# Hash attention, a dense layer and eight experts in one kernel: who stores the late rows, where some steps of the first route stand, and a one-hot made in halves

## The reference

```python
def _moe2_ref(x, w_gate, w1, w2):          # x: 1536 tokens x 512; 8 experts, hidden size 1024
    cap = N // E                           # 192 tokens for each expert
    logits = x @ w_gate
    flat = logits.flatten()
    order = np.argsort(-flat)
    for idx in order:
        tok, e = (int(idx) // E, int(idx) % E)
        if assigned[tok] >= 0 or counts[e] >= cap:
            continue
        assigned[tok] = e
        counts[e] += 1
    for e in range(E):
        mask = assigned == e
        h = np.maximum(x[mask] @ w1[e], 0.0)
        out[mask] = h @ w2[e]
```

## Time and profile before

| | us |
|---|---|
| median of 3 runs | 779.58 (777.39 to 780.97) |
| the profiled execution | 779.81 |
| its span | 778.1 |
| around the span | 1.7 |
| mean granted clock of TensorE | 0.993 of full |

### The profile page before, as it was taken

One profiled execution on the slowest core, in us unless ns is written; L12 is line 12 of the kernel. 1 busy time (PEld: TensorE's weight loads), 2 busy tenths in 40 slices (PEclk: granted clock), 3 DMA queues, 4 the chain that ended last, 5 costly groups with the idle time before them and its releaser, 6 DMA issues. The chain is left out here.

```text
span 778.1 us, 13713 instructions
## 1 busy us (share of the span) xinstructions
PE 763.2 (98%) x4537; PEld 693.0 (89%) x4537; DVE 441.7 (57%) x1103; ACT 392.7 (50%) x695; POOL 397.3 (51%) x326
## 2 busy tenths in 40 slices
PE   8999999999999999999999999999899999999996
PEld 6889898988988899999999999997699999999996
DVE  8576666756664348768766667645554455454000
ACT  3677767777676655665665666540112122122221
POOL 5677777777687587576567777530110020011111
PEclk9999999999999999999999999999799999999999
DMA  7676667666536020010010001000644645464731
GB/s 162 145 174 149 144 160 172 143 142 155 149 77 184 1 109 0 0 42 0 0 42 1 0 0 41 1 1 29 228 150 137 230 154 177 186 231 161 250 130 42
DMA packets 44548, 83.61 MB, mean 107 GB/s; under 512 B 17256, under 2 KB 17256, under 8 KB 43728
## 3 DMA queue, kind: packets, MB, share of 16 engines
q1 hardware_dynamic: 42288, 76.68, 35.0%
q0 software_dynamic: 2048, 6.29, 2.4%
q10 hardware_dynamic: 160, 0.00, 0.0%
HBM read 56.64 MB, written 6.29 MB: 81 GB/s over the span
## 5 line engine op out<-in xcount | busy, mean ns | idle before, releaser
L361 POOL TENSOR_TENSOR pt_lo<-pt,pt_hi 128x768 fp32r<-128x768 f32 x64 | 117.7, 1844 | 51.6 <-ACT pt_hi L498 44.2
L995 PE MATMUL banks<-xt_hi,split_parts 128*128 128x384 f32 (+1 forms) x512 | 141.2, 337 | 0.2 <-POOL split_parts L1019 0.2
L1019 POOL TENSOR_TENSOR split_parts<-w_in_sb,split_parts 128x512 fp32r<-128x512 f32 x64 | 84.5, 1320 | 73.8 <-ACT split_parts L1012 72.6
L491 ACT ACTIVATE pt<-banks 128x768 f32<-128x768 f32 x96 | 78.1, 813 | 65.7 <-PE banks L768 55.4
L1384 PE MATMUL banks<-split_parts,h_hi 128*128 128x512 f32 x342 | 106.6, 392 | 0.0
L612 DVE TENSOR_REDUCE mx<-banks 128x1 f32<-128x768 f32 x96 | 90.5, 957 | 23.0 <-PE banks L796 19.0
L995 PEld LDWEIGHTS banks<-xt_hi,split_parts 128*128 128x128 f32 x512 | 93.5, 188 | 3.7 <-issue 0.9
L1961 PE MATMUL banks<-x_cols,w_in_sb 128*128 128x192 f32 x512 | 95.3, 339 | 0.0
L1975 PE MATMUL banks<-expert_hidden,w_out_sb 128*128 128x192 f32 x512 | 92.2, 332 | 0.0
L1961 PEld LDWEIGHTS banks<-x_cols,w_in_sb 128*128 128x128 f32 x512 | 84.7, 196 | 2.3 <-issue 0.8
L995 PE MATMUL banks<-xt_lo,split_parts 128*128 128x384 f32 (+1 forms) x256 | 86.1, 336 | 0.0
(11 more groups left out here) (282 smaller groups left out, 1452.1 us busy)
## 6 DMA issues: line engine op xcount, KB each, us to landing
w_out_sb<-in_moe_w SPq DMA_DIRECT2D x8, 2048.0 KB, 9.5
w_in_sb<-in_moe_w SPq DMA_DIRECT2D x7, 2048.0 KB
w_in_sb<-in_moe_w_in SPq DMA_DIRECT2D x8, 512.0 KB, 6.7
w_out_sb<-in_moe_w_out SPq DMA_DIRECT2D x8, 512.0 KB, 5.3
w_out_sb<-in_k SPq DMA_DIRECT2D x16, 192.0 KB, 3.9
w_out_sb<-in_q SPq DMA_DIRECT2D x16, 192.0 KB, 4.0
v_raw<-in_v SPq DMA_DIRECT2D x16, 192.0 KB, 3.7
ka<-split_parts SPq DMA_DIRECT2D x16, 192.0 KB, 3.0
```

The costliest lines, as they stand in the source:

```text
L361: pool.tensor_tensor(pt_lo[x % 2][:], pt[j % 2][:], pt_hi[x % 2][:].bitcast(fp32), ALU.subtract).then_inc(los, 1)
L491: act.activation(halves(pt[j % 2]), both(ST), ACT.Exp, scale=SCALE).then_inc(ex, 1)
L995: last = pe.matmul(PB[i][:, 0:HALF], w_[:, k, :], x_[:, xs], start=n == 0, stop=n == 3 * DT - 1)
L1019: pool.tensor_tensor(wil[i], in_view(f), wih[i].bitcast(fp32), ALU.subtract).then_inc(wils, 1)
```

## The change

- The three late tiles are stored by ScalarE itself, from its own DMA queue, right behind the eviction of each; SyncE no longer issues them.
- In the route, two steps of VectorE (the ties in `members_and_ties`, and the first update of `waiting`) move from ahead of the counts to behind them; the step on `open_or_filled` moves one place up; `tie_taken` stands beside `slots`, and the second update of `waiting` beside `slot_placed`.
- In route 0 `row_onehot` is made in two halves of six columns each. The first raises `half_list`, the second `asked`, with no drain behind it. TensorE starts on the list with `half_list` and waits for `asked` ahead of its seventh matmul.

```diff
+        w1_rest, half_list = sem("w1_rest"), sem("half_list")
...
-            for t in range(CT):
-                sp.wait_ge(y_tile, t + 1)
-                at = (CHUNKS - 1) * HALF + t * P
-                sp.dma_start(y_rows[at:at + P, :], last_rows[t]).then_inc(stored, 16)
...
                 act.wait_ge(row_tile, t + 1)
                 act.activation(last_rows[t], PB[2 + t][:], ACT.Copy).then_inc(y_tile, 1)
+                act.wait_ge(y_tile, t + 1)
+                at = (CHUNKS - 1) * HALF + t * P
+                act.dma_start(y_rows[at:at + P, :], last_rows[t]).then_inc(stored, 16)
...
                 dve.tensor_tensor(mem[:, 0], mem[:, 0], bgt[:, 1], ALU.add)
-                dve.tensor_tensor(mem[:, 1], bgt[:, 0], bgt[:, 1], ALU.subtract)
-                dve.drain()
-                dve.tensor_tensor(alive[:], alive[:], below[:], ALU.mult)
                 dve.wait_ge(answered, step(2 * NL))
...
+                dve.tensor_tensor(mem[:, 1], bgt[:, 0], bgt[:, 1], ALU.subtract)
+                dve.drain()
+                dve.tensor_reduce(fmax[:], few[:], AX.X, ALU.max)
                 dve.tensor_tensor(cap[:], cap[:], cnt[:, 1], ALU.subtract)
-                dve.drain()
-                dve.tensor_reduce(fmax[:], few[:], AX.X, ALU.max)
+                dve.tensor_tensor(alive[:], alive[:], below[:], ALU.mult)
                 dve.drain()
...
                 dve.tensor_tensor(mem_e[:], mem[:], es[:].unsqueeze(1).unsqueeze(1).broadcast_to([P, 2, NT, E]), ALU.mult)
+                dve.tensor_scalar(openness[:], es[:], -2.0, 1.0, ALU.mult, ALU.add)
                 dve.drain()
                 dve.tensor_reduce(gm[:], mem_e[:], AX.X, ALU.max)
-                dve.tensor_scalar(openness[:], es[:], -2.0, 1.0, ALU.mult, ALU.add)
...
-                dve.drain()
-                rows_and_columns(places)
+                dve.scalar_tensor_tensor(vt[:], places[:, 1], float(CAP), gm[:, 1], ALU.is_lt, ALU.mult)
+                dve.drain()
+                rows_and_columns(True, not past(s, 1))
...
                 dve.drain()
+                if in_halves:
+
+                    dve.tensor_tensor(oh[:, 0:CH, EARLY], row[:, EARLY].unsqueeze(1).broadcast_to([P, CH, NT // 2]),
+                                      iota_j[:, 0:CH, EARLY], ALU.is_equal).then_inc(half_list, 1)
+                    dve.tensor_tensor(oh[:, 0:CH, LATE], row[:, LATE].unsqueeze(1).broadcast_to([P, CH, NT // 2]),
+                                      iota_j[:, 0:CH, LATE], ALU.is_equal).then_inc(asked, 1)
+                    return
...
                 for t in range(NT):
+                    if t == NT // 2 and not past(s, 1):
+                        pe.wait_ge(asked, STEPS)
...
                     pe.wait_ge(first_half, k // 2 + 1)
+                elif k == STEPS - 1 and not past(s, 1):
+                    pe.wait_ge(half_list, 1)
```

More of the change, by code:

```diff
@@ L1559, in experts @@
             sem(n) for n in ("asked", "answered", "e_ready", "list_ready", "w1_in0", "w1_in1", "w2_in0", "w2_in1", "gathered0", "gathered1", "xtp", "xts", "ehid", "ehs", "ecol", "ecs", "erow", "ogs", "scattered", "sp_steps", "psteps", "padded"))
-        w1_rest = sem("w1_rest")
+        w1_rest, half_list = sem("w1_rest"), sem("half_list")
         late_rows, row_tile, last_logits = late
@@ L1782, in route @@
                     dve.scalar_tensor_tensor(few[:], cnt[:, 0], float(CAP), pref[:], ALU.is_ge, ALU.mult)
-                dve.tensor_tensor(cap[:], cap[:], cnt[:, 1], ALU.subtract)
+                dve.tensor_tensor(mem[:, 1], bgt[:, 0], bgt[:, 1], ALU.subtract)
                 dve.drain()
                 dve.tensor_reduce(fmax[:], few[:], AX.X, ALU.max)
+                dve.tensor_tensor(cap[:], cap[:], cnt[:, 1], ALU.subtract)
+                dve.tensor_tensor(alive[:], alive[:], below[:], ALU.mult)
                 dve.drain()
@@ L1805, in route, with rows_and_columns @@
                 dve.scalar_tensor_tensor(slots[:], places, -NOSLOT, gm[:], ALU.add, ALU.mult)
+                dve.scalar_tensor_tensor(vt[:], places[:, 1], float(CAP), gm[:, 1], ALU.is_lt, ALU.mult)
                 dve.drain()
-                rows_and_columns(places)
+                rows_and_columns(True, not past(s, 1))
                 if more:
                     choose()
-            def rows_and_columns(places=None):
+            def rows_and_columns(ties=False, in_halves=False):
                 dve.tensor_tensor(placed[:], slots[:, 0], slots[:, 1], ALU.add)
-                if places is not None:
-                    dve.scalar_tensor_tensor(vt[:], places[:, 1], float(CAP), gm[:, 1], ALU.is_lt, ALU.mult)
+                if ties:
+                    dve.tensor_tensor(alive[:], alive[:], vt[:], ALU.subtract)
                 dve.drain()
@@ L1821, in rows_and_columns @@
                 dve.scalar_tensor_tensor(row[:], back_by[:], NOSLOT, placed[:], ALU.add, ALU.add)
-                if places is not None:
-                    dve.tensor_tensor(alive[:], alive[:], vt[:], ALU.subtract)
                 dve.tensor_tensor(ids_c[:], ids[:].unsqueeze(2).broadcast_to([P, NT, 2, 2]),
```

## The result

| | before | after |
|---|---|---|
| median of 8 runs, us | 778.89 (777.39 to 780.97) | 781.57 (780.82 to 782.39) |
| profiled execution, us | 779.81 | 781.47 |
| its span, us | 778.1 | 779.7 |
| mean granted clock | 0.993 | 0.990 |

The changed kernel is slower: the ratio is 1.0036, with a 95% interval of 1.0023 to 1.005, or 2.7 us by the medians. That is inside the 0.5% that the prediction called no change, but the interval doesn't hold 1, and the forecast was 0.2 us faster. Of all the executions in this document one is slow and left out of its ratio: 837.15 us at a mean granted clock of 0.855, in the first experiment.

A forecast was written before the change was run, and what follows sets the result against it. TensorE, busy 763.2 of 778.1 us, was taken as the bound, with gain only at the layers' switch through VectorE's route 1: 779.81 less 0.24 is 779.57, on the median's footing 779.3 us; range 776.0 to 781.4.

The forecast's parts named there:

- the one on the late rows: Late stores on ScalarE: third lands at 548.7, first weights leave 2.4 us earlier, sum unchanged if it lands by 549.7.
- sharing half and half: Third late store and first weights under way together: equal sharing delays the 2 us store by 1 us at most, to 549.7.
- rival 2: Third late store waits behind the first weights, transposes start at 557.4 instead of 555.58, time 781.4 us; chance 0.10.
- The sentence in the prediction on interleaving: DMA at the late stores: transfers started on several engines interleave on the same 16 DMA engines; only issuing time is saved.
- Nobody waits for these weights: First expert weights on SyncE: issued 2.4 us earlier without gain; before, they landed at 553.0 and expert 0 began at 558.20.
- The slack: Third late store before the gather: it may land 0.65 us later than GpSimd could use it, at 549.7, before delaying transposes.
- ScalarE's issue: Late stores issued by ScalarE: 0.59 us each against SyncE's 0.32, costing nothing since ScalarE idles 2.90 us before `token_list`.
- VectorE's sum: Switch between the layers: VectorE begins route 1 0.24 us earlier, `expert_id` 0.16 us earlier; the 0.24 kept at the transposes.
- every round of that route is a wait of TensorE for VectorE, so nothing in between eats it: Route 1 up to the transposes: VectorE's 0.24 us earlier start arrives there in full.
- What would show it: Signs in the profile after, among them `expert_id` 0.15 us early and transposes directly behind the comparison without idle for the gather.
- Rival 1: Slow stretch around 554 to 566 us: TensorE's clock doesn't fall, saving 3.3 us, time 776.0 us; chance 0.12.
- The longer slow stretch: Around the switch the lower clock lasts longer, each us costing at most 0.36; 5 us more give 781.1; chance 0.10.

The follow-up runs named there:

- the first experiment: The changed kernel with the three late stores back on SyncE's queue, VectorE's moved steps and the halves kept: 779.54 us, ratio 1.0002 to the kernel before.
- The half load: The changed kernel with only 0.5 MB of the first 1 MB weight load issued early, the rest after the late rows landed: 780.13 us, ratio 1.0002.

## Why the prediction was wrong

**The step that failed** is the one on the late rows: "sharing half and half costs a 2 us store 1 us at most, 549.7, just on the edge", and the landing at 548.7 on which the forecast rested. The store didn't share. It landed at 551.41, 2.7 us behind the forecast and 1.7 behind that edge, because nearly all of the load issued 1.05 us ahead of it (0.97 of 1.05 MB) was through before the store's first packet moved. I had a bound for this (552.6, too late by the full 2.0 us added behind the load's landing) and the right mechanism as rival 2, with 1.8 us for its price (measured 2.0 at the transposes, 1.9 in time at full clock), and gave it a chance of 0.10. Nothing in the rows spoke for equal sharing: no row showed two transfers under way at once, and I took the milder of two unknowns for the likelier. The sentence in the prediction on interleaving (the Trainium skill, DMA: Bandwidth & Descriptors, "Issuing engines are not separate DMA queues") is borne out where it says that another engine's queue brings no engines of its own. The interleaving that it speaks of is in this trace only in the last 0.6 us of the load. That a store so interleaved would get its turn early was my reading, and the first packets at 0.8, 1.5 and 3.4 us behind 0, 0.5 and 1 MB contradict it.

**"Nobody waits for these weights"** was right, and that is the point: 2.5 us of an earlier start for a load with 5 us of slack were paid for with the one transfer that had 0.65 us.

**The slack** was right. I put the decisive landing at 549.7, 3.3 us after an issue at 546.41. The half load gives exactly 3.3, and its transposes just don't wait.

**ScalarE's issue** was mis-sized: 0.33 us, like SyncE's, not 0.59. It changed nothing.

**VectorE's sum** (0.24 us): the terms up to the choice held, even too low (0.30 gained at `best` against 0.24; `expert_id` 0.18 against 0.16). A good part of the 0.30 was lost behind that point in a stall that the sum didn't have. At the transposes 0.16 us (13.13 against 12.97 in the two kernels with longer fillers on one chip) to 0.18 us (13.12 against 12.94 without them) are left, and "every round of that route is a wait of TensorE for VectorE, so nothing in between eats it" looked at the wrong engine.

**What would show it**: the prediction named the idle time of the transposes that ends with the gather as the mark of rival 2, and that mark is there, 2.12 us long.

**Rival 1's price** held: 3.3 us for the kept clock and 776.0 as the time; measured 2.7 us (the kernel before without and with the longer fillers, 779.48 and 776.76) to 3.2 us (779.54 and 776.32, in two comparisons), and 776.3 to 776.5 for the time. The rule of the Trainium skill (TensorE: Matmul & The Clock Gate, "Terms"), by which the slow stretch would have cost an estimated 5.1 us, overstates it here. One reading was loose: ten matmuls in 1.73 us at full clock and two in 0.93 at half are no factor of two, but 2.7 for each. Like against like bears it out better: two take 0.56 us at full clock (with the longer fillers) against 0.93, four take 0.90 against 1.63.

**The longer slow stretch** of the changed kernel (13.7 us instead of 10.3) is not what the wait costs. Its additional part lies ahead of expert 0. From the start of expert 0 on, 5.7 us at the lower clock are left (560.26 to some 565.9), where it was 6.9, and by the prediction's 0.36 us for each that gives back 0.4 of the 2.06 us by which expert 0 starts later. Some 1.6 us remain, and the profiled executions are 1.7 us apart (781.47 and 779.81).

**Why the medians are 2.7 us apart** when the wait is worth 1.9 less some 0.2 for VectorE is a matter of which executions are compared. All eight of the changed kernel have a mean granted clock of 0.990 to 0.992 and average 781.6. The executions of the kernel before with 0.991 or 0.992 average 779.8 to 780.1 in the three sets beside the experiments, 1.6 to 1.8 us less; in those sets 28 of 76 executions have a higher clock, and most of them are faster. Whether the changed kernel has such executions more seldom, eight don't tell: with all stores on one queue and a wait as long (2.07 us), four of ten had 0.993 to 0.995 and took 779.3 to 780.2.

**The range** ended at 781.4 for the very case that came, and 781.57 was measured. It took rival 2's price of 1.8 us, which was right, and had no width left around it for the scatter of the runs.

## What to carry to other kernels

When a transfer is freed from a queue, ask which transfers it will now stand in front of: a large load that nobody waited for, issued 1 us ahead of a small store on the critical path, held that store until it was nearly through itself, on the same queue or on another. The order in a queue, even an accidental one, can be what protects the path, so put an explicit order in its place before taking it away. A gap ahead of a dense stretch can cost twice, as the wait and again as clock, if the clock was still full when the gap began; look up when it fell before putting it to a wait's account. Filling the gaps here with idle matmuls was worth 3 us, more than ten times what reordering VectorE brought, and made the runs steady enough that 0.2 us could just be told.

## What the runs showed of the hardware

- A 256 KB store landed 2.0 us after its issue with nothing ahead, 3.3 us with 0.5 MB issued 1.04 us ahead, 4.9 to 5.3 us with 1 MB issued about 1 us ahead, on SyncE's queue as on ScalarE's, and 4.5 us on GpSimd's with 1.3 us between the issues. The store's bytes themselves wait: its first packet moved 0.8, 1.5 and 3.4 us after its issue behind nothing, 0.5 and 1 MB. Why the engines served them in this order is open.
- VectorE stood idle 0.27 to 0.28 us ahead of its fourth instruction of route 1's choice in the kernels with the old order, and 0.42 to 0.43 us in all kernels with the moved steps, with nothing in the profile that it waited for. The cause is open.
- The clock fell at 552.3 in the changed kernel, behind 1.6 us of idle time ahead of route 1's first comparison and 3 us before the wait for the gather; in the kernel before, which has no such wait, it fell at 554.9, in the 0.73 us of idle time ahead of the second comparison; with the longer fillers and the wait, at 559.4, behind 2.14 us of idle time.
- Of 30 executions of the kernel before, the two with a mean granted clock of 0.998 took 776.2 and 776.6 us; those at 0.991 to 0.993 took 777.7 to 780.4.
